# Reading the moving operands of all matmuls from their last column to their first, in a gated scan followed by a two-layer network on one core

## The reference

```python
sig = 1.0 / (1.0 + np.exp(-f_logit))
f = lower_bound + (1.0 - lower_bound) * sig          # x, f_logit: 2 x 6080 x 256
for t in range(S):
    h = f[:, t] * h + (1.0 - f[:, t]) * x[:, t]
    y[:, t] = h
hidden = y.reshape(12160, 256) @ w_in                # 256 x 2048
g = np.maximum(hidden, 0.0) ** 2
out = g @ w_out                                      # 2048 x 256
```

## Time and profile before

| | |
|---|---|
| device time, median of 3 runs | 988.72 us (988.69 to 988.76) |
| the profiled execution's own time | 988.59 us |
| its span, first to last instruction | 986.5 us |
| TensorE busy | 982.4 us, 100% of the span, 4,388 matmuls |
| weight loads busy (beside the matmuls) | 818.7 us, 83% |
| VectorE busy | 731.8 us, 74% |
| ScalarE busy | 697.4 us, 71% |
| GpSimd busy | 50.3 us, 5% |
| mean granted TensorE clock | 1.00 of full speed |

### The profile page before, as it was taken

One profiled execution on the slowest core, in us unless ns is written; L12 is line 12 of the kernel. 1 busy time (PEld: TensorE's weight loads), 2 busy tenths in 40 slices (PEclk: granted clock), 3 DMA queues, 4 the chain that ended last, 5 costly groups with the idle time before them and its releaser, 6 DMA issues.

```text
span 986.5 us, 12612 instructions
## 1 busy us (share of the span) xinstructions
PE 982.4 (100%) x4388; PEld 818.7 (83%) x4388; DVE 731.8 (74%) x940; ACT 697.4 (71%) x925; POOL 50.3 (5%) x50
## 2 busy tenths in 40 slices
PE   9999999999999999999999999999999999999998
PEld 7998888888888888888888888888888888888887
DVE  6997886876877687688688778768768767876545
ACT  8977766766776776676677677677667767766665
POOL 2682000000000000000000000000000000000000
PEclk9999999999999999999999999999999999999999
DMA  9003011002101201100210210110111021001001
GB/s 330 1 15 109 0 44 64 22 1 86 43 1 48 80 0 43 64 21 16 69 43 0 77 51 0 43 64 21 42 43 43 0 85 43 1 1 43 1 1 43
DMA packets 22158, 41.96 MB, mean 43 GB/s; under 512 B 1520, under 2 KB 3056, under 8 KB 22128
## 3 DMA queue, kind: packets, MB, share of 16 engines
q1 hardware_dynamic: 21984, 41.43, 12.1%
q10 hardware_dynamic: 144, 0.13, 0.0%
HBM read 29.11 MB, written 12.45 MB: 42 GB/s over the span
## 4 chain that ended last, share of the span: by engine, by line
PE 100%; DVE 0%; POOL 0%; issue 0%; DVEq 0%; POOLq 0%
PE out_ps L927 52%; PE hidden_ps L912 42%; PE hidden_ps L953 4%; PE out_ps L947 1%; PE out_ps L953 1%; PE out_ps L937 0%; POOL zeros L888 0%; DVE result L848 0%; DVE result L853 0%; DVE result L850 0%; DVEq L852 0%; DVEq L847 0%; POOLq L1204 0%
## 5 line engine op out<-in xcount | busy, mean ns | idle before, releaser
L927 PE MATMUL out_ps<-g_hi,w_out_lo 128*128 128x512 f32 (+1 forms) x760 | 294.2, 387 | 0.0
L927 PE MATMUL out_ps<-g_lo,w_out_hi 128*128 128x512 f32 (+1 forms) x760 | 294.2, 387 | 0.0
L927 PE MATMUL out_ps<-g_hi,w_out_hi 128*128 128x512 f32 (+1 forms) x760 | 294.1, 387 | 0.0
L700 DVE TENSOR_TENSOR g_lo<-h,g_hi 128x1024 fp32r<-128x1024 f32 (+1 forms) x189 | 231.9, 1227 | 64.2 <-ACT g_hi L416 61.0
L409 ACT ACTIVATE h<-h 128x1024 f32<-128x1024 f32 (+1 forms) x189 | 199.2, 1054 | 3.2
L927 PEld LDWEIGHTS out_ps<-g_hi,w_out_hi 128*128 128x128 f32 x760 | 142.7, 188 | 28.3
L927 PEld LDWEIGHTS out_ps<-g_lo,w_out_hi 128*128 128x128 f32 x760 | 142.7, 188 | 28.2
L927 PEld LDWEIGHTS out_ps<-g_hi,w_out_lo 128*128 128x128 f32 x760 | 142.7, 188 | 28.0
L912 PE MATMUL hidden_ps<-sums_hi,wc_hi 128*128 128x512 f32 x352 | 137.0, 389 | 0.0
L912 PE MATMUL hidden_ps<-sums_lo,wc_hi 128*128 128x512 f32 x352 | 137.0, 389 | 0.0
L912 PE MATMUL hidden_ps<-sums_hi,wc_lo 128*128 128x512 f32 x352 | 136.9, 389 | 0.0
(11 more groups left out here) (114 smaller groups left out, 1054.6 us busy)
## 6 DMA issues: line engine op xcount, KB each, us to landing
f_in<-f_logit_t SPq DMA_DIRECT2D x22, 512.0 KB, 4.6
x_in<-x_t SPq DMA_DIRECT2D x22, 512.0 KB, 4.5
out_t<-result SPq DMA_DIRECT2D x20, 512.0 KB, 3.1
w_out_raw<-weights SPq DMA_DIRECT2D x8, 256.0 KB, 6.7
w_in_raw<-weights SPq DMA_DIRECT2D x5, 256.0 KB, 6.5
out_t<-result SPq DMA_DIRECT2D x2, 448.0 KB, 3.0
w_in_raw<-first SPq DMA_DIRECT2D x3, 256.0 KB, 4.1
out_t<-result SPq DMA_DIRECT2D x3, 256.0 KB, 2.0
```

Source lines behind the costliest of these rows:

```text
L700: nc.vector.tensor_tensor(g_lo[b][:, :, 0:n], h_of(it, j, b), g_hi[b][:, :, 0:n].bitcast(F32), ALU.subtract).then_inc(g_ready[b], 1)
L927: mm = nc.tensor.matmul(out_ps[:, b, c, in_bank(it)], half[:, j, m, c * P:(c + 1) * P], moving[b][:, m, 0:n], start=(j == 0 and m == 0 and ...
```

## The change

All matmuls but those of zeros read their moving operand from its last column to its first: the operand's slice gets `[:, ::-1]`. The output is written from the first column to the last as before. So a tile of `h` lies turned round in time, and with it `g_hi` and `g_lo`; the second product reads these turned round again, and its output has the old order. Where only some columns of a tile are treated, the slice on the turned side is mirrored (`turned`): a part of the first tile goes to the mirrored columns of its bank, and a half of the very last product reads the mirrored columns of `g`.

```diff
 product:
-                    mm = nc.tensor.matmul(hidden_ps[:, bank, 0:n], half[:, j, w], moving,
+                    mm = nc.tensor.matmul(hidden_ps[:, bank, 0:n], half[:, j, w], moving[:, ::-1],
 second:
-                                          moving[b][:, m, 0:n], start=(j == 0 and m == 0 and k == 0),
+                                          moving[b][:, m, 0:n][:, ::-1], start=(j == 0 and m == 0 and k == 0),
 very_last_second:
+                turned = slice(N - columns.stop, N - columns.start)
-                                          moving[b][:, m, columns], start=opens and k == 0,
+                                          moving[b][:, m, turned][:, ::-1], start=opens and k == 0,
 first_part:
+                turned = slice(NARROW - columns.stop, NARROW - columns.start)
-                    mm = nc.tensor.matmul(banks[:, m, columns], half[:, j, blocks[c]],
-                                          first_block(*of, b, c)[:, columns], start=opens, stop=signal is not None,
+                    mm = nc.tensor.matmul(banks[:, m, turned], half[:, j, blocks[c]],
+                                          first_block(*of, b, c)[:, columns][:, ::-1], start=opens,
+                                          stop=signal is not None,
```

## The result

The changed kernel takes 1016.34 us (median of 4 runs, 1016.06 to 1016.80) against 988.74 us before: 1.0278 times as long, with an interval of 1.0261 to 1.0296. The forecast was no change. The profiled execution took 1016.14 us with a span of 1014.1 us, 27.6 us more than the span of before.

A forecast was written before the change was run, and what follows sets the result against it. TensorE's queue of matmuls was taken as the bound: steps summing to 976.2 us, plus a 6.6 us start and a tail. With nothing added, the forecast was the median, 988.7 us, range 986.5 to 1,047 us.

The forecast's parts named there:

- What bounds the kernel: Whole kernel: TensorE, busy 982.4 of 986.5 us, sets the time; VectorE and ScalarE wait for it.
- the sum of steps: All 4,374 turned matmuls: counts times distances between starts give 976.2 us, against 976.8 us in the trace.
- the price of zero for a downward read: Each of 4,374 matmuls: reading the moving operand downwards adds nothing, leaving 988.7 us; chance of no change 0.66.
- the nearest row: Matmul loop: 512 columns of another tile keep the same 226.7 ns step, taken as grounds for zero added.
- upper bounds: Sizes kept for extra time per matmul: 2.6 ns each, 11 us in all, or 13.3 ns each, 58 us.
- the step of -1 as such: Moving operand reads: a step of -1 might not be treated as a contiguous read; named the simplest way to be wrong.
- The gap: Each matmul: the step beyond one column a cycle, 13.3 ns at 512 columns, 12.4 at 256, 15.9 at 448.
- larger gap: Start of each matmul: downward reading costs more at the operand's end, 1,000 us at 2.6 ns, 1,047 us doubled; chance 0.14.
- Half the column rate: Moving reads: one column every second cycle, 916 us more, about 1,905 us; chance 0.15 including other losses in the columns.
- The smaller gap: Each matmul: downward reads collide less with the weight load; 960 us at half, 930 us at none; chance 0.05.
- The rule of the Trainium skill on lines of 16 bytes: SBUF reads: four columns share a line in either direction, so the time stays at 988.7 us.

The follow-up runs named there:

- The tables: Three sets of rows of 30 matmuls behind the last store of the kernel before, varying direction, place, width and weights; 226.7 ns up, 233.3 down at 512 columns.
- The third table: Kernel before plus rows of matmuls behind its last store, weights' start shifted through 256 bytes; upward 226.7 to 234.4 ns, downward 233.3, at three places 236.7.
- the first table: Kernel before plus 47 rows of matmuls behind its last store, varying direction, width, start, column step, weights and type; 512 columns took 226.7 ns up, 233.3 down.

## Why the prediction was wrong

**What bounds the kernel** was right, and the test of it too: the sum of steps is the kernel. The 27.7 us worked out from the steps of the changed kernel is its loss to 0.1 us, and nothing hid any of it.

**The step that failed** is the price of zero for a downward read. I took it from "the nearest row", the same 512 columns of other tiles at the same step, and argued that tile and block change nothing. They change nothing because they vary nothing: every moving operand here, and every block of weights, starts at the same place within 256 bytes. The tables, where that place was varied, have 226.7 to 234.4 ns for upward reads of 512 columns. A step that repeats without scatter was read as a sign that reading is no limit; it was one fortunate fit, repeated in all 3,954 matmuls of 512 columns. The measured price is 6.6 ns at 512 columns, between the 2.6 and the 13.3 ns that I had kept as upper bounds. Nor is it the step of -1 as such, which I named last as the simplest way to be wrong: with each group of 4 columns turned round in its place, the steps inside each group are -1, and the kernel takes 988.75 us. What costs in a downward read of 512 columns is the order of the 16-byte groups within 256 bytes.

**The gap** was called a fixed cost of each matmul, with the weight load lying harmlessly under the matmul before. The trace pointed elsewhere, and I used it only as a size for the larger gap: 448 columns had 15.9 ns where 512 had 13.3, which a fixed cost does not do. Moving the weights alone, by 64 bytes, moves the step by 6.6 ns. The Trainium skill (SBUF — State Buffer, Who interferes with whom) gives TensorE two read ports, one for the moving operand and one for the weight load, and calls them independent; read plainly, by that the weights' place could not change the step. The third table (226.7 against 233.3 ns) shows that it does, so the measurement decides.

**The rivals.** A larger gap, at 0.14, had the right sign, and its upper size stretched the range so far that it held the time. That is luck, since the mechanism was not this one: it was to start at the operand's end and to cost 256 columns as much as 512, and they cost nothing (119.1 before, 118.2 ns after). Half the column rate is out: the step of 512 columns grew by 6.6 ns, where it would have grown by 213. The smaller gap named the meeting of the moving read and the weight load, and dismissed it; for upward reads that was the right place to look, with the sign turned round: of all orders and places tried for float32r none was faster than the kernel before, and most lost. The rule of the Trainium skill on lines of 16 bytes (Advanced Engine Details and Errata, SBUF Cachelines), which I cited for no change, agrees with groups of 4 turned round (988.75 us), but it is silent on the order of the lines, and that cost the time here. Nor do all rows bear it out: upward reads at a step of 2 columns, two to a line, take 451.1 ns in the first table, hardly less than the 461.3 ns at a step of 4, where each column has a line of its own.

**What stays open.** For upward reads it is shown that the place of the weights changes the step, and that a start 16 bytes on costs even when the weights move alike; a rule that gives the step of each place is not. For downward reads it is not shown that the weights take part: the step is 233.3 ns with 128 or 32 columns of weights, nearly wherever they lie, and some 231 with bf16 weights. A matmul without a weight load of its own was not tried, so whether the downward order is slow by itself or through the weight load is left open. So is why 320 and 256 columns don't pay, and why blocks of 16 columns turned round in their place cost 40 ns.

## What to carry to other kernels

Where TensorE bounds a kernel and its operands are four bytes wide, the distance between matmul starts depended here on how the moving operands lie to the weights within 256 bytes and on the order in which 16-byte groups are read within 256 bytes; check it against a row with shifted addresses before calling it fixed, and keep tiles at whole multiples of 256 bytes. Padding of 32 bytes in the wrong place cost this kernel 27 us without touching an instruction. Rows that all agree are evidence only about what differs between them.

## What was not expected of the hardware

- Upward float32r reads of 512 columns step at 544 cycles at 2.4 GHz in the kernel's own layout (and with the weights 4 columns to either side of it), and at 549 to 563 at most other places; bf16 steps at 518 (215.8 ns), whichever way it is read.
- bf16 at a step of 2 columns steps at 225.8 ns, not 215.8; at a step of 4 columns at 451.6 ns, the same as float32r at a step of 2 (451.1).
- After a change of direction the steps need some matmuls to settle (232.7, 240.0, 230.8, then 233.3 ns), and a mixture can be slower than its parts: half of the matmuls turned round cost 21.5 or 23.3 us, all of them 27.6.
- No order or place tried was faster for float32r than the kernel before: 226.7 ns was the least for 512 columns in all three tables.
